# First products and cross-diagonal products of a 32-step recurrence on other 32x32 tiles of TensorE

## The reference, cut to what matters

```python
y[:, :, t] = np.einsum('bhd,bhde->bhe', rt, state)
Sa = np.einsum('bhde,bhe->bhd', state, at)
state = state * wt[:, :, None, :] - np.einsum('bhd,bhe->bhde', Sa, bt) + np.einsum('bhd,bhe->bhde', vt, kt)
```

## Time and profile before

| what | us |
|---|---|
| median of 3 runs | 1126.1 |
| lowest, highest | 1124.49, 1138.29 |
| span of the profiled execution | 1129.2 |
| TensorE matmuls busy | 1072.3 (95%) |
| TensorE weight loads busy | 917.0 (81%) |
| VectorE, ScalarE, GpSimd busy | 595.8, 397.3, 146.4 |

### The profile page before, as it was taken

One profiled execution on the slowest core, in us unless ns is written; L12 is line 12 of the kernel. 1 busy time (PEld: TensorE's weight loads), 2 busy tenths in 40 slices (PEclk: granted clock), 3 DMA queues, 4 the chain that ended last, 5 costly groups with the idle time before them and its releaser, 6 DMA issues.

```text
span 1129.2 us, 36605 instructions
## 1 busy us (share of the span) xinstructions
PE 1072.3 (95%) x16106; PEld 917.0 (81%) x16106; DVE 595.8 (53%) x1306; ACT 397.3 (35%) x782; POOL 146.4 (13%) x179
## 2 busy tenths in 40 slices
PE   2888979999999999999999999999999999999998
PEld 2777868888888887788788788888888888888887
DVE  7797786767676776667574224443223232323222
ACT  2142243344444443533343335542222222222222
POOL 6313030403122121303010000000000000000000
PEclk9977679999999999999999999999999999999999
DMA  5836363344335342434333024220201002020000
GB/s 176 252 103 151 68 129 80 82 110 123 85 75 134 89 108 62 125 90 100 64 110 79 9 91 145 80 89 1 61 1 57 5 1 61 1 61 1 24 1 23
DMA packets 133856, 87.62 MB, mean 78 GB/s; under 512 B 98274, under 2 KB 113634, under 8 KB 133700
## 3 DMA queue, kind: packets, MB, share of 16 engines
q1 hardware_dynamic: 126740, 62.85, 22.8%
q0 software_dynamic: 6960, 22.45, 6.6%
HBM read 66.39 MB, written 18.87 MB: 76 GB/s over the span
## 4 chain that ended last, share of the span: by engine, by line
PE 89%; issue 4%; DVE 3%; ACT 1%; POOL 1%; DMA 0%; SPq 0%; ACTq 0%; POOLq 0%; DVEq 0%
PE bank L808 16%; PE bank L858 12%; PE pair L858 12%; PE bank L823 4%; PE bank L878 4%; PE bank L876 4%; PE bank L877 4%; PE bank L824 4%; PE bank L825 4%; PE bank L894 3%; PE bank L783 2%; PE bank L760 2%; PE bank L774 2%; PE bank L630 2%; PE bank L828 2%
## 5 line engine op out<-in xcount | busy, mean ns | idle before, releaser
L1301 DVE TENSOR_TENSOR g_lo<-g_full,g_hi 128x512 fp32r<-128x512 f32 x168 | 125.3, 746 | 229.8 <-ACT g_hi L1064 229.6
L1064 ACT CAST g_hi<-g_full 128x512 fp32r<-128x512 f32 x168 | 104.3, 621 | 134.7 <-DVE g_full L1354 131.6
L808 PE MATMUL bank<-x_hi,w_up 128*128 128x512 f32 x480 | 134.7, 410 | 3.6 <-issue 3.6
L1057 ACT ACTIVATE g_full<-bank 128x512 f32<-128x512 f32 x96 | 57.5, 599 | 210.0 <-PE bank L808 204.7
L1256 DVE TENSOR_TENSOR t_unit<-t_unit,prod 128x126 f32<-128x126 f32 (+22 forms) x372 | 106.5, 286 | 12.8
L1252 DVE TENSOR_TENSOR prod<-t_unit,p_unit 128x126 f32<-128x126 f32 (+22 forms) x372 | 102.1, 275 | 20.1 <-DMA p_unit<-p_dram 7.0
L808 PEld LDWEIGHTS bank<-x_hi,w_up 128*128 128x128 f32 x480 | 85.4, 189 | 23.0 <-issue 4.5
L1354 DVE TENSOR_TENSOR g_full<-pair,h_sb 128x512 f32<-128x512 f32 x36 | 24.9, 692 | 112.7 <-PE pair L858 112.0
L808 PE MATMUL bank<-x_lo,w_up 128*128 128x512 f32 x288 | 82.1, 393 | 0.0
L823 PE MATMUL bank<-g_hi,w_dn 128*128 128x512 f32 x192 | 76.4, 398 | 0.4 <-DVE g_lo L1301 0.2
L824 PE MATMUL bank<-g_hi,w_dn 128*128 128x512 f32 x192 | 75.0, 391 | 0.0
(11 more groups left out here) (146 smaller groups left out, 2401.0 us busy)
## 6 DMA issues: line engine op xcount, KB each, us to landing
p_unit<-p_dram SPq DMA_DIRECT2D x48, 128.0 KB, 2.9
stage<-in_w_out POOLq DMA_DIRECT2D x7, 640.0 KB, 5.8
v_tok<-in_vT SPq DMA_DIRECT2D x12, 320.0 KB, 3.1
v_nu<-in_vN SPq DMA_DIRECT2D x24, 160.0 KB, 5.9
x<-y_sb SPq DMA_DIRECT2D x48, 80.0 KB
k_sb<-in_kF POOLq DMA_DIRECT2D x22, 160.0 KB, 3.4
v_sb<-in_vF SPq DMA_DIRECT2D x22, 160.0 KB
r_sb<-in_rF SPq DMA_DIRECT2D x22, 160.0 KB
```

Of the source, the lines that this page charges most:

```text
L808: last = nc.tensor.matmul(up_bank(m)[:], lhs, rhs, start=(e == 0), stop=(e == len(products) - 1))
L1064: nc.scalar.copy(g_hi[:, m % 2], g_full[:]).then_inc(g_hi_ready, 1)
L1301: nc.vector.tensor_tensor(g_lo[:, m % 2], g_full[:], g_hi[:, m % 2].bitcast(F32), ALU.subtract).then_inc(g_lo_ready, 1)
```

## The change

The first products of q >= 4 (four of the eight sequences of each i) are written to the lower 32 partitions of each half instead of the upper ones, and so are their scores `p_cross`; the cross products of q >= 4 read both from there. Both blocks issue q in the order 0, 4, 1, 5, 2, 6, 3, 7. `act_a` writes `p_cross` in four instructions of 32x128 instead of two of 32x256. The count of products, their sizes, the banks and all waits stay.

```diff
+        HQ = TQ // 2
+
+        def first_rows(i, q):
+
+            return upper(i) if q < HQ else lower(i)
...
-            for q in range(TQ):
-                for i in range(2):
-                    last = nc.tensor.matmul(o[upper(i), q * D:(q + 1) * D], t_sb[upper(i), c, q, 0:C],
+            for q in (x for low in range(HQ) for x in (low, low + HQ)):
+                for i in range(2):
+                    last = nc.tensor.matmul(o[first_rows(i, q), q * D:(q + 1) * D], t_sb[upper(i), c, q, 0:C],
                                             rhs_sb[upper(i), q], start=True, stop=True)
...
-            for q in range(TQ):
-                for i in range(2):
-                    last = nc.tensor.matmul(rhs_place(q)[lower(i)], p_cross[upper(i), u % 2, c, q],
-                                            u_first[upper(i), q], start=False, stop=True, skip_group_check=True)
+            for q in (x for low in range(HQ) for x in (low, low + HQ)):
+                for i in range(2):
+                    last = nc.tensor.matmul(rhs_place(q)[lower(i)], p_cross[first_rows(i, q), u % 2, c, q],
+                                            u_first[first_rows(i, q), q], start=False, stop=True,
+                                            skip_group_check=True)
...
-                last = nc.scalar.mul(p_cross[upper(i), u % 2, c], src[upper(i), :, C:L], -1.0)
+                for q in (0, HQ):
+                    last = nc.scalar.mul(p_cross[first_rows(i, q), u % 2, c, q:q + HQ],
+                                         src[upper(i), q:q + HQ, C:L], -1.0)
```

## The result

| | median us | lowest, highest | runs |
|---|---|---|---|
| before | 1129.37 | 1123.04, 1138.29 | 20 |
| after | 1125.35 | 1117.9, 3507.34 | 20 |

The ratio is 0.9957, with a 95% interval of 0.9938 to 0.9976: the change saves about 4.9 us, between 2.7 and 7.0 (slow executions, such as the one of 3507.34 us, are left out of the ratio). The sign and the likeliest case, within 2%, came out as forecast; the size did not. 8.7 us were forecast, and a little over half of that arrived. The median, 1125.35, stands 8.0 above the forecast 1117.4, outside the forecast's own range of 1113 to 1121; 3.3 of the 8.0 come from the starting point, since the three runs before had a median of 1126.1 and the twenty here have 1129.37. The profiled execution took 1121.54 us with a span of 1119.5, so 2.0 us lie around the span.

The account below looks back on a forecast made before the run. TensorE's instruction stream was taken to bound the kernel from 165 us on; 10.3 - 0.8 - 2.0 - 0.3 + 1.5 = 8.7 us, off the median 1126.1, gave 1117.4 us, range 1113 to 1121 (8 in 10: 1111 to 1129).

Parts of the forecast that it names:

- parts (1) and (2): First and cross products on four tiles in turn: 0.27 us saved a block, 10.3 us over 38 middle-stretch blocks.
- rival A: Issue-bound: eight TensorE instructions can't be fed in 36 ns, a round stays at 58; 2.3 us saved, 1123.8; chance 0.18.
- Rival B: Only one block kind gains, since tiles on the same 32 rows take turns; 3.6 us saved, 1122.5; chance 0.09.
- Rival C: Tiles within a quarter don't overlap, both blocks stay at 18 ns a matmul, evictions cost 2.3 us; 1128.4; chance 0.13.
- part (4): Four small act_a evictions on ScalarE at 260 ns each delay sn six times, -2.0 us, and -0.3 at the start.
- part (3): Three middle-stretch down products wait for g_lo, losing 0.8 us; elsewhere VectorE and ScalarE results are in time by over 0.27.
- part (6): "Issue" holes of about 1 us after long runs of small TensorE products: let stand, no term in the sum.
- part (5): The ten blocks before 165 us, some at half clock: 1.5 us saved, between 0 and 3.5.
- rival D: Before 165 us the clock falls in other places; a 10 us stretch costs about 5 us: 1122, or 1112; chance 0.10.

Follow-up runs that it names:

- tiles_only: The changed kernel with its new tiles and four score evictions, but q in the old order 0 to 7 in both blocks; 0.998 of the kernel before.
- first_in_turn: The changed kernel with the new q order only in the first products, the cross products in order 0 to 7; 0.9957 of the kernel before.
- after_fill: The changed kernel with two more identity products behind each of the ten blocks of n = 0 to 4; 0.9947 of the kernel before.
- cross_in_turn: The changed kernel with the new q order only in the cross products, the first products in order 0 to 7; 0.9958 of the kernel before.
- after_glo: The changed kernel with VectorE's six columns of the inverse at step 0 moved behind g_lo; 0.9973 of the kernel before.

## Why the prediction was right or wrong

**The block, parts (1) and (2): right, exactly.** 0.27 us a block was forecast from the period of 36 ns and the rounds of four; 0.273 was measured in both kinds, 10.4 us in the middle stretch against 10.3. A round of four in 36 ns is eight instructions at 4.5 ns each, so rival A's limit of some 7 ns an instruction isn't there; it would have given blocks of 0.65. Blocks of 0.65 did appear, in `tiles_only`, and for another reason. Rival B fell with `first_in_turn`: tiles on the same 32 rows don't take turns, which is against the rule of the Trainium skill (TensorE: Matmul & The Clock Gate, Part 3, The mechanism) that a weight load overlaps only across row groups. Nor does the floor of some 25 ns from start to start that the Trainium skill gives (the same page, Part 1, the section on the 56 ns gap) hold on several tiles: 9 ns a matmul were measured. Rival C fell with either block.

**The evictions, part (4): right.** 260 ns a piece was worked out and 263 measured; 2.0 us before `sn` was forecast and 2.08 measured, six times.

**What hides behind a late partner, part (3): the step that failed first.** The forecast took the three places where g_lo was late and lost 0.27 us at each, 0.8 in all. Measured was 1.78 us: 0.55, 0.20 and 0.40 at these three and 0.64 at a fourth, where g_lo had been in time. The window between the first products and the down product isn't only 0.27 shorter; g_lo is also later relative to it. The premise that failed is "VectorE is late by itself there". VectorE and GpSimd hinder each other where both have a tensor_tensor. The kernel after, VectorE and then GpSimd at the new wait:

```profile
514.65 1.68 DVE L1310 TENSOR_TENSOR g_lo<-g_full,g_hi 128x512 fp32r<-128x512 f32 x1
```
```profile
514.53 1.25 POOL L307 TENSOR_TENSOR a_sb<-a_sb,decay 128x512 f32<-128x512 f32 x1
```
```profile
516.39 0.50 PE L830 MATMUL bank<-g_hi,w_dn 128*128 128x512 f32 x1 [0.48 <-DVE g_lo L1310]
```

The down product waits for 514.65 + 1.68 = 516.33. At the same place before, VectorE came to it in a gap of GpSimd's:

```profile
521.14 0.68 DVE L1301 TENSOR_TENSOR g_lo<-g_full,g_hi 128x512 fp32r<-128x512 f32 x1
```
```profile
519.57 1.18 POOL L321 TENSOR_TENSOR k_sb<-k_sb,inv 128x512 f32<-128x512 f32 x1 [2.07 <-DMA k_sb<-in_kF]
521.21 1.67 POOL L311 TENSOR_TENSOR b_sb<-b_sb,inv 128x512 f32<-128x512 f32 x1 [0.47 <-DMA b_sb<-in_bF]
```

There VectorE had begun first, and it was GpSimd's instruction that took 1.67 instead of some 1.2. GpSimd's work arrives with its DMAs and VectorE's with TensorE's progress; the shorter blocks slid one against the other, and g_lo was stretched 16 times after against 13 before. Each of the 23 g_lo in the two traces that took over 0.9 us ran beside a tensor_tensor of GpSimd and ended 0.54 to 0.56 us after that one's end; of the 295 with no such neighbour none was stretched. The forecast read 1.68 us for g_lo in the earlier trace rows and took it for a given of that place, without asking why it wasn't 0.68. It also called the other two places alike, and one was not. There, before, VectorE's columns of the inverse were stretched instead, 1.2 to 1.3 us where such a one takes 0.28 alone, and g_lo itself took 0.68:

```profile
310.09 1.18 DVE L1256 TENSOR_TENSOR t_unit<-t_unit,prod 128x133 f32<-128x133 f32 x1
311.19 0.68 DVE L1301 TENSOR_TENSOR g_lo<-g_full,g_hi 128x512 fp32r<-128x512 f32 x1
```

That it is chance of phase, and not the shorter block, which made g_lo later by just so much isn't excluded: `tiles_only` has it late at none of these four places, and at one other. Part (3) also said that all other results were in time by over 0.27 us. `rhs_sb` wasn't: in windows 4, 6 and 8 its copy stands on ScalarE behind the new block's `x_hi`, and 3 x 0.21 us went there (the other handovers of that kind gave 0.19 back, hence 0.44 in the table). In part this step named the right mechanism and mis-sized it, 0.8 for 2.2 in all.

**The holes, part (6): failed by taking two things for one.** "Let stand" was taken for the holes at counts 193 and 194 too; they came out 0.65 us better, and that is luck. The larger "issue" entry, before the up products, was the wait for `x_lo`, and it grew by 0.8 us. The text had the sentence that applies: if a hole ends at a time fixed before the block, the saving in it is lost. It could have been found in the earlier trace rows by looking for what had just ended on any engine 0.1 us before each resumption.

**The start, part (5): not borne out, and not settled.** 1.5 us was taken and none is seen: `after_fill` put more back than the ten blocks had shed and lost nothing that shows. The ratio alone, 4.9 us within 2.2, leaves room for 1.5 beside the 5.3 of the late part only at its far end. The profiled pair shows 4.4 us ahead of 165 us, but with 24 us less at half clock after, which is rival D's mechanism; from one execution of each kernel the two can't be parted.

**The sum.** 10.38 - 2.08 - 1.78 - 0.80 - 0.44 - 0.64 (small distances between groups, 0.38 + 0.26) + 0.65 (the boundary holes, 1.10 + 0.33 - 0.78) = 5.29 us in the middle stretch, with nothing counted before it, against 8.7 forecast. The excess of the forecast is 1.5 for the start, 1.0 and 0.4 in part (3), 0.8 in part (6), 0.6 of small distances between groups that no part named, less the 0.3 it had charged at the start and the 0.65 of luck. The table is of one execution of each kernel, and in the ratio the saving is only known to 2 us: the terms for waits and holes would come out otherwise in another pair, and how much of them is chance stays open. The block times and the 2.08 before `sn` recur block by block.

## What to carry to other kernels

Small fp32 products on tiles of 32x32 ran here at the pace of one tile, so spreading a block over four tiles instead of two nearly halved it, whether the tiles share rows or columns. Count then, for each engine that feeds TensorE, how much slack each handover has, since every one with less than the saving gives it back, and more than half of the loss here lay in handovers that the profile called "issue" or that looked fixed. An "issue" wait that recurs once in a period of the program is likely a data wait: look for a result that ended 0.1 us before it. Keep instructions that only copy out of the way of those that release a bank.

## What was not expected of the hardware

- Tiles work independently of each other: with the second pair issued after the first, a second rhythm of starts sets in 178 ns into the block, which I read as the second pair ahead of earlier-issued matmuls on the other tiles, and the block takes 457 ns from first to last start in place of 566. Four 32x32 tiles in turn keep 36 ns a round, 9 ns a matmul and 4.5 ns an instruction.
- Mostly in runs of small products, TensorE stops for 0.7 to 2.2 us (in `after_fill` up to 3.1) at counts of 193 or 194 modulo 256 recorded instructions, 1.2 to 1.6 us after an instruction packet of 16 KB has landed, and adding 48 instructions early changed which products are hit. The ratio went from 0.9902 [0.9869, 0.9935] to 0.9842 [0.981, 0.9873], 0.6 points, with intervals that just touch; 2.5 us of it are seen behind the start.
- A g_lo, VectorE's tensor_tensor of 128x512, that runs beside one of GpSimd lasts up to 2.51 us instead of 0.68 (12 of 22 in the kernel after over 0.9), and one of GpSimd that begins just behind VectorE's 1.67 instead of some 1.2. Mostly the one that began later is the one stretched, but not in the row of 464.05, which took 2.51 us: GpSimd was issuing DMAs when it began, and a tensor_tensor of GpSimd followed 0.75 us later and ended 0.56 us ahead of it:

```profile
463.74 1.06 POOL L426 DMA_DIRECT2D a_sb<-in_aF  x2
464.80 1.20 POOL L327 TENSOR_TENSOR k_sb<-k_sb,inv 128x512 f32<-128x512 f32 x1
```

- A stop of about 2 us in TensorE's work can be followed by products at half clock, 0.42 us apart instead of 0.23: it was so behind 2.16 us in `cross_in_turn`, and not behind 2.00 us in `after_glo`.
